# An attention chunk's k^T v as two matmuls of 64 stationary columns instead of one of 128

## The chip, the core and the metric

The kernel runs on one core of a Trainium2 chip. The metric is the device time of one execution in microseconds; the time before is the median of three executions. The engines in the text are TensorE (PE, with its weight loads as PEld), VectorE (DVE), ScalarE (ACT), GpSimdE (POOL) and the queues that issue DMAs (SP above all).

## The reference: what is computed

Three layers follow one another, on a batch of 4, 8 heads, 768 tokens and a head width of 48, all in fp32. The first is an attention with a decaying state, a 48 x 48 matrix for each head:

```
for t in range(S):
    state = alpha[:, :, t, :, None] * state + np.einsum('bhd,bhe->bhde', k[:, :, t], v[:, :, t])
    y[:, :, t] = np.einsum('bhd,bhde->bhe', q[:, :, t], state)
```

Then a token mixer and a channel mixer (`h = relu(x^T w_tok1) w_tok2`, `u = x + h^T`, `h2 = relu(u w_ch1) w_ch2`, result `u + h2`), and last a second channel mix with a receptance gate (`k = relu(xk w_k)`, `v = k*k w_v`, result `sigmoid(xr w_r) * v`).

## The kernel before

The attention is done in chunks of 128 tokens. A batch has 6 chunks and 4 pairs of heads, so 24 attention steps; the two heads of a pair lie in partitions 0 to 63 and 64 to 127, 48 of each 64 in use. In a step, TensorE transposes q, k and alpha (`transposes`, L500); VectorE scans alpha to the running product `decay` and to `suffix`, and scales q and k by them (`scans`, `scale_qk`); ScalarE and VectorE split the scaled operands into a high and a low part; TensorE transposes the scaled k (L514) and multiplies k by q for the scores (L518 in the first round, L522 later); VectorE masks the scores (`mask`, L922). `attention_out` then makes the chunk's output `y_ps` from the masked scores and v (L538), adds the part that comes from the state (L541), and, in all chunks but the last, computes k^T v into `kv_ps` (L544). ScalarE takes `y_ps` out (`high_x`, L745), and VectorE's `outputs` writes the new state from `kv_ps` (L939 in the first chunk, L941 later), and then the low part of x (L944). GpSimdE multiplies the old state by the chunk's whole decay (`carry_state`, L421).

The state of a pair is one tile of 128 x 96: head 0's 48 x 48 in its upper left part, head 1's in its lower right one, and zeros elsewhere (set once by a memset), so that one matmul (L541) serves both heads. v is kept zero padded in the same way: `vt3[vb][:, p, h, :]` has 96 columns, head h's 48 in their place and 48 of zeros. `kv_ps` is columns 128 to 223 of the PSUM bank in which `y_ps` has columns 0 to 95.

A matmul of fp32 operands is carried out as two pairs of instructions, each a weight load and a matmul (in the trace, a `matmul` of fp32 stands twice); a matmul of operands of type fp32r is one pair. The k^T v is of fp32; the mixer's matmuls (L617, L633) are of fp32r, three of them for each product.

Around the attention the work runs in rounds. Round 0 has only the attention of batch 0, in a pipeline of three steps' depth, beside the loading and splitting of the mixers' weights on ScalarE and GpSimdE. Rounds 1 to 3 (a loop on each engine) have 28 slots each: the attention of batch r, and interleaved with it, in the order of the code, the mixers of batch r - 1: two slots for the first token matmul, two for the second, then 24 channel-mixer units of nine L617 and nine L633 matmuls. In slot s `attention_out` is done for step s - 2, so slots 2 to 21 have a k^T v each, the last 18 of them beside a channel-mixer unit. After them come the mixers of batch 3 alone and the last layer. There is no scheduler: each engine executes its instructions in the order in which they are written, and semaphores hold it back. `y_done` tells ScalarE that a step's `attention_out` is through, `xhi_ready` tells VectorE that ScalarE has taken y, `state_ready` goes to GpSimdE and to TensorE's next chunk.

Of the kernel before, what the change touches and what calls it, by code (L numbers as in the profile page):

```python
# [13 lines left out]
def attention_mixer_channel_mix(nc, q, k, v, alpha, w_tok1, w_tok2, w_ch1, w_ch2,  # L14
# [4 lines left out]
    ALU = mybir.AluOpType  # L19
# [3 lines left out]
    B, H, S, D = q.shape  # L23
# [6 lines left out]
    DP = 64  # L30
# [21 lines left out]
    with ctx:  # L52
        def sb(name, shape, dt=F32):
            return ctx.enter_context(nc.sbuf_tensor(name, shape, dt))
# [29 lines left out]
        def wr_w(n, kt):  # L84
# [23 lines left out]
        kdt = relu_k[:, :, 2 * P:3 * P]  # L108
        state = sb("state", [P, NP, W2])
        state_d = sb("state_d", [P, 4, W2])  # L110
# [14 lines left out]
             for half, o in ((0, 0), (0, H * DP), (1, 0))]]  # L125
        qbd = free_words[1][:, H * DP:H * DP + 4 * P].rearrange("p (n t) -> p n t", n=2)
        vt3 = vt + [mixed[:, :, :].rearrange("p a t -> p (a t)")[:, 0:NP * 2 * W2]
                    .rearrange("p (a h e) -> p a h e", a=NP, h=2)]
# [24 lines left out]
        def y_kv(r, i):  # L153

            b_y = bank[6] if is_first(r) and i % 2 else bank[2]
            return b_y[:, 0:W2], b_y[:, P:P + W2]
# [100 lines left out]
        def chunk_buffer(r, c):  # L257


            if is_first(r):  # L260
                return c % 3, c // 3 + 1
            return c % 2, NC // 2 * (r - 1) + c // 2 + 1 + NC // 3
# [4 lines left out]
        def step(i):  # L267
            return i // NP, i % NP
# [115 lines left out]
        def _(pool):  # L384
# [24 lines left out]
            def split_lo(n):  # L409

                _, dst, off = PIECES[n]
                rows, cols = piece_size(n)
                pool.wait_ge(w_hi_ready, n + 1)
                nc.gpsimd.tensor_tensor(dst[1][:, off:off + rows * cols], staging(n)[0],
                                        dst[0][:, off:off + rows * cols], ALU.subtract).then_inc(w_lo_ready, 1)
# [34 lines left out]
            for n in range(NEARLY, NMIX):  # L450

                _, dst, off = PIECES[n]
                rows, cols = piece_size(n)
                raw, loaded, value = staging(n)
                pool.wait_ge(loaded, value)
                nc.gpsimd.tensor_copy(dst[0][:, off:off + rows * cols], raw).then_inc(w_hi_ready, 1)
                split_lo(n)
# [19 lines left out]
        def _(pe):  # L477
            PASSES = ((0, 0), (0, 1), (1, 0))

            def v_pair(vb, p):  # L480

                return vt3[vb][:, p, :, :].rearrange("p h e -> p (h e)").rearrange(
                    "p (n d) -> p n d", d=D)[:, 0:4:3, :]

            def transposes(r, i):
                c, p = step(i)
                qb, loads = chunk_buffer(r, c)
                if is_first(r) and i == 0:
                    pe.wait_ge(consts_g, 5)
                    pe.wait_ge(pair_loaded, 48)  # L490
                if is_first(r) and i == 1:
                    pe.wait_ge(consts_g, 15)
                if i % NP == (1 if is_first(r) and i < NP else 0):
                    pe.wait_ge(qka_loaded[qb], 48 * loads)
                if not isinstance(r, int):
                    pe.wait_ge(kd_ready, STEPS * r + i)
                elif i >= 2:
                    pe.wait_ge(kd_ready, i - 1)
                for n, dst in enumerate(transposed_qka(r, i)):
                    mm = nc.tensor.transpose(  # L500
                        dst, qka3[qb][n][:, 2 * p:2 * p + 2, :].rearrange("p h d -> p (h d)"), ident[:, :])
                mm.then_inc(tr_done, 1)
# [22 lines left out]
            def attention_out(r, i):  # L525
                c, p = step(i)
                pe.wait_ge(am_ready, STEPS * r + i + 1)
                vb, loads = chunk_buffer(r, c)
                pe.wait_ge(v_loaded[vb], 32 * loads)
                y_ps, kv_ps = y_kv(r, i)  # L530
                if not isinstance(r, int):
                    pe.wait_ge(xlo_ready, STEPS * r + i)
                elif i >= 2:
                    pe.wait_ge(xlo_ready, i - 1)
                if c > 0:
                    pe.wait_ge(state_ready, NST * r + i - NP + 1)
                for h in range(2):
                    mm = nc.tensor.matmul(y_ps, am[:, i % 2, h * P:(h + 1) * P], vt3[vb][:, p, h, :],  # L538
                                          start=(h == 0), stop=(h == 1 and c == 0))
                if c > 0:  # L540
                    mm = nc.tensor.matmul(y_ps, qd[:, i % 4, :], state[:, p, :], start=False, stop=True)  # L541
                if c < NC - 1:
                    pe.wait_ge(kdt_ready, NST * r + i + 1)
                    mm = nc.tensor.matmul(kv_ps, kdt[:, i % 2, :],  # L544
                                          v_pair(vb, p),
                                          start=True, stop=True)
                mm.then_inc(y_done, 1)

            def attention_part(r, s):
                tr, sc, yo = steps_of(r, s)  # L550
                if not is_first(r) and yo is not None:
                    attention_out(r, yo)
                if sc is not None:
                    attention_scores(r, sc)
                if tr is not None:
                    transposes(r, tr)
                if is_first(r) and yo is not None:
                    attention_out(r, yo)
# [162 lines left out]
        def _(act):  # L721
            def split_hi(n):
                _, dst, off = PIECES[n]
                rows, cols = piece_size(n)
                raw, loaded, value = staging(n)
                act.wait_ge(loaded, value)
                nc.scalar.activation(dst[0][:, off:off + rows * cols], raw, ACT.Copy).then_inc(w_hi_ready, 1)
# [139 lines left out]
        def _(dve):  # L867
# [58 lines left out]
            def outputs(r, i):  # L926
                c, p = step(i)
                G = STEPS * r + i
                y_ps, kv_ps = y_kv(r, i)
                dve.wait_ge(xhi_ready, G + 1)  # L930
                if 0 < c < NC - 1:
                    dve.wait_ge(state_d_ready, NSP * r + i - NP + 1)
                if c < NC - 1:
                    for h in range(2):
                        lanes = slice(h * DP, (h + 1) * DP)
                        kv = kv_ps[lanes, h * D:(h + 1) * D]
                        own = state[lanes, p, h * D:(h + 1) * D]
                        if c == 0:
                            ins = nc.vector.tensor_copy(own, kv)  # L939
                        else:  # L940
                            ins = nc.vector.tensor_tensor(own, kv, state_d[lanes, i % 4, h * D:(h + 1) * D], ALU.add)  # L941
                    ins.then_inc(state_ready, 1)
                xs = slice(p * W2, (p + 1) * W2)
                nc.vector.tensor_tensor(x[1][:, c, xs], y_ps, x[0][:, c, xs], ALU.subtract).then_inc(xlo_ready, 1)  # L944

            def attention_part(r, s):
                tr, sc, yo = steps_of(r, s)
                if is_first(r):
                    if sc is not None:
                        mask(r, sc)  # L950
                elif yo is not None:
                    outputs(r, yo)
                if tr is not None:
                    scans(r, tr)
                    scale_qk(r, tr)
                if is_first(r):
                    if yo is not None:
                        outputs(r, yo)
                else:
                    if sc is not None:  # L960
                        mask(r, sc)
                    if tr is not None:
                        split_low(r, tr)
# [139 lines left out]
```

## Time and profile before

| | |
|---|---|
| time, median of 3 executions | 812.43 us (810.9 to 812.52) |
| span of the profiled execution | 811.5 us |
| PE, PEld busy | 779.0 us (96%), 765.0 us (94%) |
| DVE, ACT, POOL busy | 492.4 us (61%), 332.8 us (41%), 103.9 us (13%) |
| mean granted TensorE clock | 0.989 of full speed |

The profile describes one execution; its span goes from the first instruction to the last. PE's matmuls are pipelined, and the duration given for one is from its start to its modelled end, so that durations overlap: how fast a stream of matmuls runs is read from the distance between starts. The busy shares are means over stretches with different limits: round 0 (up to about 59 us), rounds 1 to 3 (to about 470 us) and the rest, in which the change has no part.

### The profile page before, as it was taken

Reading aid. Unit: us, or ns where it says so; the run is one execution under the profiler, and the core shown is the slowest. Engines: PE = TensorE matmul, PEld = TensorE weight load, DVE = VectorE, ACT = ScalarE, POOL = GpSimd, SP = SyncE. Lnnn points to the kernel's source line nnn. Section 1 sums busy time; section 2 is a strip of 40 time slices with the busy share of each in tenths; the row PEclk is TensorE's granted clock in tenths of the full one; section 3 lists DMA queues with packets and bytes.
Section 4 is the critical chain, followed back from the end, with each engine's and each line's share of the span. In section 5 each row is a group of like instructions: output and inputs, shape, how many; then the busy total and the mean of one; then the engine's idle time right before and its main releaser. Section 6 shows DMA issues by size and latency. Waiting matters only on the chain.

```text
span 811.5 us, 14781 instructions
## 1 busy us (share of the span) xinstructions
PE 779.0 (96%) x4864; PEld 765.0 (94%) x4864; DVE 492.4 (61%) x1463; ACT 332.8 (41%) x848; POOL 103.9 (13%) x146
## 2 busy tenths in 40 slices
PE   6998999999999999899999999999699999999998
PEld 5887999998899999899999999999699999999998
DVE  7987777872677776367787522224835744744751
ACT  4773434331333433143334213125445644743741
POOL 2564000201000110100020013003200000000000
PEclk9999999999999999999999999999899999999999
DMA  9973223330132232112232003200101101101000
GB/s 189 202 171 64 40 42 52 66 57 21 40 51 40 41 69 40 41 30 40 48 50 74 1 30 99 93 30 16 45 29 50 39 29 49 39 29 49 10 29 29
DMA packets 114895, 43.88 MB, mean 54 GB/s; under 512 B 102160, under 2 KB 112016, under 8 KB 114832
## 3 DMA queue, kind: packets, MB, share of 16 engines
q1 hardware_dynamic: 113680, 38.36, 22.8%
q0 software_dynamic: 1152, 4.72, 1.6%
q8 instruction: 35, 0.57, 0.3%
q14 instruction: 28, 0.23, 0.1%
HBM read 33.63 MB, written 9.44 MB: 53 GB/s over the span
## 4 chain that ended last, share of the span: by engine, by line
PE 81%; DVE 8%; issue 5%; ACT 3%; POOL 1%; SPq 1%; DMA 1%; DVEq 0%; ACTq 0%; POOLq 0%
PE bank L633 17%; PE bank L617 17%; PE bank L699 12%; PE bank L677 12%; PE bank L686 5%; PE bank L538 3%; PE bank L522 3%; PE bank L597 3%; PE bank L500 2%; PE bank L603 2%; PE bank L541 2%; PE bank L571 2%; PE bank L544 1%; ACT qs_hi L756 1%; DVE decay L893 1%
## 5 line engine op out<-in xcount | busy, mean ns | idle before, releaser
L756 ACT ACTIVATE qs_hi<-qd,rlast 64x128 fp32r<-64x128 f32 x144 | 57.6, 400 | 145.2 <-DVE qd L903 143.4
L969 DVE SCALAR_TENSOR_TENSOR hid_lo<-bank,hid_hi 128x384 fp32r<-128x384 f32 x96 | 53.1, 553 | 71.4 <-ACT hid_hi L765 71.4
L765 ACT ACTIVATE hid_hi<-bank 128x384 fp32r<-128x384 f32 x96 | 46.5, 485 | 71.7 <-PE bank L617 71.7
L912 DVE SCALAR_TENSOR_TENSOR qs_lo<-qd,rlast,qs_hi 64x128 fp32r<-64x128 f32 x144 | 57.3, 398 | 27.9 <-ACT qs_hi L756 25.6
L845 ACT ACTIVATE relu_k<-bank 128x384 f32<-128x384 f32 x64 | 31.5, 492 | 102.3 <-PE bank L677 77.4
L617 PE MATMUL bank<-u_hi,wch_hi 128*128 128x384 f32 x288 | 71.1, 355 | 0.0
L617 PE MATMUL bank<-u_lo,wch_hi 128*128 128x384 f32 x288 | 66.0, 336 | 0.0
L617 PE MATMUL bank<-u_hi,wch_lo 128*128 128x384 f32 x288 | 65.6, 335 | 0.0
L633 PE MATMUL bank<-hid_lo,wch_hi 128*128 128x384 f32 x288 | 65.5, 334 | 0.0
L633 PE MATMUL bank<-hid_hi,wch_hi 128*128 128x384 f32 x288 | 65.4, 334 | 0.0
L633 PE MATMUL bank<-hid_hi,wch_lo 128*128 128x384 f32 x288 | 65.4, 334 | 0.0
L1072 DVE TENSOR_TENSOR x_half<-bank,x_half 128x384 f32<-128x384 f32 x24 | 13.4, 558 | 77.2 <-PE bank L699 77.2
L1059 DVE TENSOR_TENSOR relu_k<-relu_k 128x384 f32<-128x384 f32 x64 | 43.4, 678 | 27.6 <-ACT relu_k L845 24.8
L421 POOL TENSOR_TENSOR state_d<-state,decay 128x96 f32<-128x96 f32 x64 | 21.9, 345 | 266.0 <-DVE decay L893 266.0
L745 ACT ACTIVATE x_hi<-bank 128x96 fp32r<-128x96 f32 x96 | 24.0, 250 | 73.2 <-PE bank L544 56.7
L500 PE MATMUL bank<-ident,qka 128*128 128x128 f32 x264 | 45.4, 283 | 8.0 <-POOL causal L401 4.1
L538 PE MATMUL bank<-vt,relu_k 128*128 128x96 f32 x352 | 51.8, 270 | 0.7 <-DVE relu_k L922 0.7
L677 PE MATMUL bank<-x_hi,wtok_hi 128*128 128x384 f32 x192 | 44.8, 341 | 7.5 <-ACT relu_k L845 7.5
L538 PEld LDWEIGHTS bank<-vt,relu_k 128*128 128x128 f32 x352 | 50.5, 192 | 1.6 <-DVE relu_k L922 1.6
L617 PEld LDWEIGHTS bank<-u_lo,wch_hi 128*128 128x128 f32 x288 | 51.6, 188 | 0.0
L617 PEld LDWEIGHTS bank<-u_hi,wch_lo 128*128 128x128 f32 x288 | 51.6, 188 | 0.0
L633 PEld LDWEIGHTS bank<-hid_hi,wch_hi 128*128 128x128 f32 x288 | 51.2, 188 | 0.1
(126 smaller groups left out, 1855.5 us busy)
## 6 DMA issues: line engine op xcount, KB each, us to landing
w_raw<-in_moe_w_ch SPq DMA_DIRECT2D x12, 384.0 KB, 4.1
x_scratch<-x_half POOLq DMA_DIRECT2D x8, 576.0 KB, 3.5
out<-x_half SPq DMA_DIRECT2D x24, 192.0 KB, 1.9
vt<-in_v SPq DMA_DIRECT2D x44, 96.0 KB, 2.4
qka<-in_q SPq DMA_DIRECT2D x21, 192.0 KB, 3.2
qka<-in_k SPq DMA_DIRECT2D x21, 192.0 KB, 4.0
qka<-in_alpha SPq DMA_DIRECT2D x21, 192.0 KB, 4.2
qka<-x_scratch SPq DMA_DIRECT2D x4, 577.5 KB, 3.9
```

Of the source, the lines that this page charges most:

```text
L500: mm = nc.tensor.transpose(dst, qka3[qb][n][:, 2 * p:2 * p + 2, :].rearrange("p h d -> p (h d)"), ident[:, :])
L538: mm = nc.tensor.matmul(y_ps, am[:, i % 2, h * P:(h + 1) * P], vt3[vb][:, p, h, :], start=(h == 0), stop=(h == 1 and c == 0))
L617: mm = nc.tensor.matmul(dst, ch1_w(a, n % KC, jj), u[c][:, n % KC, half * HT:(half + 1) * HT], start=(n == 0), stop=(n == 3 * KC - 1))
L633: mm = nc.tensor.matmul(b_acc[m][:, 0:HT], ch2_w(a, jj, m), hid[c][:, j % HJ, :], start=(jj == 0 and n == 0), stop=(jj == NJ - 1 and n == 2))
L677: mm = nc.tensor.matmul(dst, wk_w(a, n % KC, j), mix_out[0][c][:, half, n % KC, :], start=(n == 0), stop=(n == 3 * KC - 1))
L686: mm = nc.tensor.matmul(b_acc[m][:, 0:DM], mix_out[1][a][:, half, n % KC, m * P:(m + 1) * P], wr_w(c, n % KC), start=(n == 0), stop=(n == ...
L699: mm = nc.tensor.matmul(bank[m][:, 0:DM], k2[a][:, n % NF, m * P:(m + 1) * P], wv_w(c, n % NF), start=(n == 0), stop=(n == 3 * NF - 1))
L756: nc.scalar.activation(dst[lanes, h * P:(h + 1) * P], qd[lanes, i % 4, :], ACT.Copy, scale=rlast[lanes, i % 4:i % 4 + 1])\
L765: nc.scalar.activation(dst, b_ring[t % 2][:, 0:HT], func).then_inc(tile_hi, 1)
L912: nc.vector.scalar_tensor_tensor(qs[1][lanes, cols], qd[lanes, i % 4, :], rlast[lanes, i % 4:i % 4 + 1], qs[0][lanes, cols], ALU.mult, ALU ...
L969: ins = nc.vector.scalar_tensor_tensor(dst, src, 0.0, hi, ALU.max, ALU.subtract)
L1059: nc.vector.tensor_tensor(relu_k[:, j % 2, :], relu_k[:, j % 2, :], relu_k[:, j % 2, :], ALU.mult).then_inc(k2_ready, 1)
```

## The change

On TensorE the k^T v of a pair, one matmul with 128 stationary columns (both heads' k) and the 96 columns of v that hold values, becomes two matmuls. Each has the 64 stationary columns of one head, streams that head's zero padded 96 columns of v, and writes its half of the PSUM partitions. On VectorE the two instructions that copied each head's 64 x 48 part into the state become one on the whole 128 x 96 tile, since the other parts are now zeros. Nothing else changes: the semaphores and their counts, and the order of all else, stay.

```diff
-            def v_pair(vb, p):
-
-                return vt3[vb][:, p, :, :].rearrange("p h e -> p (h e)").rearrange(
-                    "p (n d) -> p n d", d=D)[:, 0:4:3, :]
-
...
                 if c < NC - 1:
                     pe.wait_ge(kdt_ready, NST * r + i + 1)
-                    mm = nc.tensor.matmul(kv_ps, kdt[:, i % 2, :],
-                                          v_pair(vb, p),
-                                          start=True, stop=True)
+                    for h in range(2):
+                        lanes = slice(h * DP, (h + 1) * DP)
+                        mm = nc.tensor.matmul(kv_ps[lanes, :], kdt[:, i % 2, lanes], vt3[vb][:, p, h, :],
+                                              start=True, stop=True)
                 mm.then_inc(y_done, 1)
...
                 if c < NC - 1:
-                    for h in range(2):
-                        lanes = slice(h * DP, (h + 1) * DP)
-                        kv = kv_ps[lanes, h * D:(h + 1) * D]
-                        own = state[lanes, p, h * D:(h + 1) * D]
-                        if c == 0:
-                            ins = nc.vector.tensor_copy(own, kv)
-                        else:
-                            ins = nc.vector.tensor_tensor(own, kv, state_d[lanes, i % 4, h * D:(h + 1) * D], ALU.add)
+                    if c == 0:
+                        ins = nc.vector.tensor_copy(state[:, p, :], kv_ps)
+                    else:
+                        ins = nc.vector.tensor_tensor(state[:, p, :], kv_ps, state_d[:, i % 4, :], ALU.add)
                     ins.then_inc(state_ready, 1)
```

TensorE, a slot of the loop of rounds 1 to 3, from the end of a channel-mixer unit to the next transposes; before (an fp32 matmul stands once here; `relu_k` is the storage of the transposed k and `vt` that of v):

```order
L633 MATMUL bank<-hid_lo,wch_hi 128x384 x3
L538 MATMUL bank<-vt,relu_k 128x96 x2
L541 MATMUL bank<-state,qd 128x96
L543 REGISTER_ALU
L544 MATMUL bank<-vt,relu_k 128x96
L506 REGISTER_ALU
L514 MATMUL bank<-ident,kd 128x128
```

and the same place now:

```order
L629 MATMUL bank<-hid_lo,wch_hi 128x384 x3
L533 MATMUL bank<-vt,relu_k 128x96 x2
L536 MATMUL bank<-state,qd 128x96
L538 REGISTER_ALU
L541 MATMUL bank<-vt,relu_k 64x96 x2
L501 REGISTER_ALU
L509 MATMUL bank<-ident,kd 128x128
```

One matmul of 128 stationary columns became two of 64, between two neighbours of 128; line numbers are smaller since the helper is gone.

VectorE, a step of round 0, from the scaling of k to the next scan; before:

```order
L905 TENSOR_TENSOR kd<-bank,suffix 128x128
L941 TENSOR_TENSOR state<-bank,state_d 64x48 x2
L944 TENSOR_TENSOR x_lo<-bank,x_hi 128x96
L922 COPY_PREDICATED relu_k<-causal,bank 128x256
L893 SCALAR_TENSOR_TENSOR decay<-bank,zeros 128x128
```

and now:

```order
L901 TENSOR_TENSOR kd<-bank,suffix 128x128
L933 TENSOR_TENSOR state<-bank,state_d 128x96
L936 TENSOR_TENSOR x_lo<-bank,x_hi 128x96
L918 COPY_PREDICATED relu_k<-causal,bank 128x256
L889 SCALAR_TENSOR_TENSOR decay<-bank,zeros 128x128
```

Two instructions of 64 x 48 became one of 128 x 96, of the same size as the one behind it.

## Rows read from the trace of the kernel before

**Rows 1.** The page: busy time, clock in 40 slices, chain by engine.
```profile
PE 779.0 (96%) x4864; PEld 765.0 (94%) x4864; DVE 492.4 (61%) x1463; ACT 332.8 (41%) x848; POOL 103.9 (13%) x146
...
PE 81%; DVE 8%; issue 5%; ACT 3%; POOL 1%; SPq 1%; DMA 1%; DVEq 0%; ACTq 0%; POOLq 0%
```

**Rows 2.** PE timeline, one slot of round 1: start us, us, engine, line, what.
```profile
157.99 0.58 PE L538 MATMUL bank<-vt,relu_k 128*128 128x96 f32 x4
...
159.33 0.49 PE L500 MATMUL bank<-ident,qka 128*128 128x128 f32 x3
159.57 0.77 PE L617 MATMUL bank<-u_hi,wch_hi 128*128 128x384 f32 x3
...
162.78 0.47 PE L538 MATMUL bank<-vt,relu_k 128*128 128x96 f32 x3
```

**Rows 3.** Chain of waits, 138 to 150 us: start us, us, what.
```profile
138.31 0.24 PE bank L544 x2
...
138.57 0.26 ACT x_hi L745
...
144.27 0.19 DVE state L941
...
149.27 0.62 PE bank L522 x3
```

**Rows 4.** Line L544 alone: count, duration ns min/median/max, first and last start.
```profile
L544 PE MATMUL bank<-vt,relu_k x152: 275/275/421, 12.8 to 443.1; 128*128 128x96 f32 x152
...
L544 PE MATMUL bank<-mixed,relu_k x8: 275/275/275, 28.9 to 34.8; 128*128 128x96 f32 x8
```

**Rows 5.** PE timeline around one k^T v of round 1.
```profile
153.19 0.58 PE L538 MATMUL bank<-vt,relu_k 128*128 128x96 f32 x4
153.60 0.39 PE L541 MATMUL bank<-state,qd 128*128 128x96 f32 x2
153.83 0.39 PE L544 MATMUL bank<-vt,relu_k 128*128 128x96 f32 x2
154.05 0.27 PE L514 MATMUL bank<-ident,kd 128*128 128x128 f32 x1
```

**Rows 6.** The weight loads at the same place.
```profile
153.52 0.30 PEld L541 LDWEIGHTS bank<-state,qd 128*128 128x128 f32 x2
153.74 0.30 PEld L544 LDWEIGHTS bank<-vt,relu_k 128*128 128x128 f32 x2
```

**Rows 7.** PE timeline, round 0: two fp32 matmuls of 256 columns, then three transposes.
```profile
27.38 0.27 PE L514 MATMUL bank<-ident,kd 128*128 128x128 f32 x1
27.49 0.60 PE L518 MATMUL bank<-x_half,kd 128*128 128x256 f32 x2
27.92 0.49 PE L500 MATMUL bank<-ident,x_half 128*128 128x128 f32 x3
28.25 0.25 PE L538 MATMUL bank<-mixed,relu_k 128*128 128x96 f32 x1
```

**Rows 8.** DVE timeline, one step of round 0.
```profile
28.36 0.41 DVE L941 TENSOR_TENSOR state<-bank,state_d 64x48 f32<-64x48 f32 x2
28.81 0.26 DVE L944 TENSOR_TENSOR x_lo<-bank,x_hi 128x96 fp32r<-128x96 f32 x1
...
30.39 0.41 DVE L941 TENSOR_TENSOR state<-bank,state_d 64x48 f32<-64x48 f32 x2
```

**Rows 9.** Chain of waits in round 0: first and last state, and a POOL piece.
```profile
16.24 0.04 DVE state L939
...
36.16 0.81 POOL wch_lo L414
...
52.77 0.19 DVE state L941
```

**Rows 10.** DVE timeline, the two slots of round 2 without a channel-mixer unit.
```profile
212.17 0.56 DVE L971 TENSOR_TENSOR u_lo<-bank,u_hi 128x384 fp32r<-128x384 f32 x1 [1.21 <-ACT u_hi L765]
212.65 0.41 DVE L939 COPY state<-bank 64x48 f32<-64x48 f32 x2
213.09 0.26 DVE L944 TENSOR_TENSOR x_lo<-bank,x_hi 128x96 fp32r<-128x96 f32 x1
...
219.75 0.41 DVE L939 COPY state<-bank 64x48 f32<-64x48 f32 x2
```

## The prediction, made before the changed kernel ran

> **What bounds the kernel now.** I read the page first. TensorE is 96% busy and holds 81% of the chain of work that ended last; VectorE has 8% of it [rows 1]. Those are means, so next I read stretches with the timeline. In rounds 1 to 3 a slot with a channel-mixer unit repeats every 4.79 us (L538 at 157.99 and again at 162.78), and TensorE starts one matmul after another in it [rows 2]: there every nanosecond added between two matmuls is paid. The chain shows the exceptions. Once a round, from 138.57 to 149.27 us in round 1, it leaves TensorE and runs over ScalarE and VectorE, until L522 goes on [rows 3]; TensorE idles at its end. The two slots ahead of the channel-mixer units are led by the hand-over TensorE, ScalarE, VectorE [rows 10]. In round 0 the chain lies mostly on VectorE, with pieces on GpSimdE in the middle, as at 36.16 us [rows 9]; a step takes 30.39 - 28.36 = 2.03 us [rows 8].
>
> The changed lines work from 12.8 to 443.1 us and 160 matmul records belong to them, so 80 k^T v [rows 4]: 20 in round 0 and 20 in each of rounds 1 to 3. Of the 20 of a round, 18 stand beside a channel-mixer unit; two of these lie in the stretch from 138.57 to 149.27 us (or its like in rounds 2 and 3), where VectorE leads and TensorE has time [rows 3]. That leaves 3 x 16 = 48 on TensorE's path.
>
> **What a k^T v costs TensorE now.** From the first L541 matmul (153.60) to L514 (154.05) there are four intervals in 0.45 us, 0.112 us each [rows 5]. What sets it? Two fp32 matmuls of 256 columns take 27.92 - 27.49 = 0.43 us, 0.215 each [rows 7], so 0.84 ns for a column and 0.081 us for 96: shorter than 0.112. I conclude that streams of 96 columns are paced by the loading of 128 stationary columns, not by the stream. From the second L541 to L514 it is three intervals, 0.335 us.
>
> **What it costs afterwards.** Four matmuls instead of two, each still streaming 96 columns, so 0.082 each, with a weight load half as wide, which I take to be hidden (half of the 0.112 or less). Then the matmul ahead of the first, and the first three of them, have 0.082 us each, and the last, with a load of 128 columns behind it, 0.112: 0.440 us. That is +0.105, if nothing else happens.
>
> Something else may: every matmul in this trace has a 128 x 128 stationary operand, and the change alternates with 128 x 64 ones, in and out again, 80 times. No row shows what that costs. The low end is nothing, or even a gain, if the two heads, which lie in different columns of the array, stream side by side: only three intervals of 0.082 and one of 0.112 remain, 0.358, or +0.02. The high end is that the array empties first: the whole 0.275 us duration of the matmul in flight [rows 4] and a load that hides under nothing. A load stands 0.08 us ahead of its matmul (153.52 to 153.60, and 153.74 to 153.83) [rows 5, 6]; I take 0.06 for 64 columns. Going in, 0.275 + 0.06 = 0.335; three of 0.082; going out, 0.275 + 0.083 = 0.358; sum 0.939, or +0.60.
>
> I take a value between, the nearest that rows give a mechanism for: the next load can't be pulled ahead over a change of shape, but waits only until the stream before it is through. In 0.082 + 0.06 = 0.142, inside 0.246, out 0.082 + 0.083 = 0.165: 0.553 against 0.335, **+0.22 us** for each k^T v.
>
> Here the Trainium skill speaks against the change: "TensorEngine Tiling (Array Packing)", Key Properties, says that changing the tiling mode drains TensorE, though changing the tile does not. No run here shows it; by that rule the sum would lie at my value or above it.
>
> **What VectorE gains.** The two 64 x 48 instructions take 28.81 - 28.36 = 0.45 us until the next one starts; the next is 128 x 96 from the same bank and takes 0.26 [rows 8]. The new instruction has that shape, so -0.19 us. It counts where VectorE leads:
> - Rounds 1 to 3: two states in the stretch of rows 3, two in the slots of rows 10, so 12 x 0.19 = -2.3 us. In the latter, `y_done` comes some tenths later, while VectorE still has L971 and ScalarE its u_hi; I count nothing for it, and at most 0.2 us for each of 6 at the high end.
> - Round 0: twelve steps of the chain have a state of VectorE (first at 16.24, last at 52.77); in seven GpSimdE's splitting of weights leads, which doesn't change [rows 9]. VectorE's step would fall from 2.03 to 1.84. But TensorE is not idle: a step has L518 0.43, three transposes 0.33, L514 0.11 [rows 7], L538 0.41, L541 and L544 0.22 each [rows 5], in all 1.72 us; with 0.22 more 1.94, so it becomes the bound. Gain 0.09 x 12 = -1.1 us.
>
> In all other slots VectorE's saving hides behind TensorE's channel-mixer matmuls. POOL's `carry_state` and the DMAs see the same order and semaphores; nothing new waits. `y_done`, on the last of the four matmuls, comes at worst some tenths later; ScalarE and VectorE have idle time there.
>
> **Sum.** 48 x 0.22 = +10.6; -2.3; -1.1: +7.2 us, so a span of 818.7. The median of the runs is 812.43 and the profiled span 811.5, 0.9 less; the forecast in the measure of the runs is **819.6 us**.
>
> **Rivals.** What this kernel's measurement can tell from no change is about 0.2%, 1.6 us: faster is below 810.8, slower above 814.0.
> - *Side by side, no price for the change of shape* (+0.02): 48 x 0.02 = 1.0, -2.3, and round 0 stays VectorE's at 1.84 a step, 12 x 0.19 = -2.3: -3.6, or 808.8. For it: the heads' columns and PSUM partitions are disjoint. Against: each head's high and low pass still follow one another, and each needs a load. The skill's "TensorE: Matmul & The Clock Gate", Part 3, says that matmuls in different column groups run concurrently, starting about 4 ns apart. No row here shows it; by that rule, alone, the time is this one.
> - *Side by side, but with the forecast's price at the two borders*: 0.142 + 0.164 + 0.165 = 0.471, +0.136. 48 x 0.136 = 6.5, -2.3, -2.0: +2.2, or 814.6.
> - *One after another, no price at the borders* (+0.105): 48 x 0.105 = 5.0, -2.3, -2.3: +0.4, or 812.9.
> - *The array empties at each border* (+0.60): 48 x 0.60 = 28.8; in round 0 TensorE's step becomes 1.72 + 0.60 = 2.32, +0.29 for all 20, 5.8; the late `y_done` 1.2; -2.3: +33.5, or 846. For it: nothing in the trace says that a matmul of another shape may enter behind one in flight.
>
> The first rival is the one on the other side. It decides where a k^T v costs TensorE less than 0.05 us more: below that VectorE's -4.6 us outweighs 48 x 0.05 by more than the measurement's uncertainty.
>
> **Chances.** Forecast 0.36; emptied array 0.22 (with the values between it and the forecast); side by side without price 0.20; one after another without price 0.12; side by side with price 0.10. The likeliest gives the time, 819.6; its own range, with a border price between 0.03 and 0.10 us, is 816 to 825. The range for 8 in 10 leaves out a little on either side: 808 to 847. Faster by over 0.2%: 0.22, the side-by-side case and a little of the next. Within 0.2%: 0.13. Slower: 0.65.
>
> **What would show it.** In the slot of rows 2 the distance from L538 to L538 should be 5.01 us instead of 4.79; the emptied array would show 5.39, side by side 4.81. From the second state matmul to the transpose of k I expect 0.55 instead of 0.335 us, with a gap ahead of the first and behind the last of the four, and their starts 0.08 apart; starts of the two heads within a few nanoseconds would show them side by side. VectorE's state should be 80 instructions of about 0.25 us in place of 160 of 0.2, and its step in round 0 down to 1.94, with VectorE now waiting for TensorE there. The forecast fails if the weight loads of 64 columns are not hidden or the shape change costs more than 0.1 us a border; it fails the other way if the heads overlap. It also fails if VectorE's new instruction takes as long as the two (0.41): then 3.4 us of gain are gone, and the forecast's case becomes 823.

## The result and the profile after

The changed kernel takes 824.78 us (median of 4 runs, 823.62 to 825.48), the kernel before in the same session 812.03 us (810.9 to 812.52). The ratio is 1.0156, with a 95% interval of 1.014 to 1.0172: slower by 12.7 us. The forecast was 819.6 us, slower by 7.2; the direction held, and the time lies at the upper edge of the forecast's own range (816 to 825).

The page of the changed kernel, busy time and chain, answers to [rows 1]:

```profile
PE 794.0 (96%) x5024; PEld 765.9 (93%) x5024; DVE 479.8 (58%) x1383; ACT 332.6 (40%) x848; POOL 104.0 (13%) x146
...
PE 88%; DVE 4%; issue 4%; ACT 2%; DMA 1%; SPq 1%; DVEq 0%; ACTq 0%
```

TensorE has 160 pairs of instructions more, VectorE 80 instructions less, and VectorE's share of the chain went from 8% to 4%. The span is 823.5 us instead of 811.5.

The PE timeline of one slot of round 1 (start us, us, engine, line, what), against [rows 2, 5]:

```profile
157.29 0.58 PE L533 MATMUL bank<-vt,relu_k 128*128 128x96 f32 x4
157.71 0.39 PE L536 MATMUL bank<-state,qd 128*128 128x96 f32 x2
158.03 0.39 PE L541 MATMUL bank<-vt,relu_k 128*64 128x96 f32 x4
158.34 0.33 PE L509 MATMUL bank<-ident,kd 128*128 128x128 f32 x1
158.43 0.36 PE L517 MATMUL bank<-qs_hi,ks_hi 128*128 128x256 f32 x1
...
162.33 0.58 PE L533 MATMUL bank<-vt,relu_k 128*128 128x96 f32 x4
```

The slot has become 162.33 - 157.29 = 5.04 us long, from 4.79. From the first state matmul to the transpose of k it is 0.63 us (157.71 to 158.34) instead of 0.45, and the score matmul follows the transpose after 0.09 instead of 0.03: +0.18 and +0.06 make the +0.24. The 128*64 in the third row is the new stationary shape.

A narrow window of the same timeline shows how the four matmuls of a k^T v stand to each other:

```profile
157.82 0.28 PE L536 MATMUL bank<-state,qd 128*128 128x96 f32 x1
158.03 0.30 PE L541 MATMUL bank<-vt,relu_k 128*64 128x96 f32 x2
```

By 158.10 two of the four have started, both ended within 0.30 us. In the trace's single records the four start at 0, 7, 134 and 140 ns: two and two nearly at once. The first comes 0.205 us after the matmul ahead of it, where two matmuls of equal shape are 0.112 apart; the transpose comes 0.177 us after the last. The weight loads of the same place show why there is a gap:

```profile
157.63 0.30 PEld L536 LDWEIGHTS bank<-state,qd 128*128 128x128 f32 x2
158.03 0.20 PEld L541 LDWEIGHTS bank<-vt,relu_k 128*64 128x64 f32 x4
158.34 0.14 PEld L509 LDWEIGHTS bank<-ident,kd 128*128 128x128 f32 x1
```

Before, the loads of L541 and L544 stood 0.08 us ahead of their matmuls and under the matmul before [rows 5, 6]. Now the first load of the new shape starts at 158.03, when its matmul is shown to start too, 0.20 us after the last matmul of the old shape (157.82); and the first load of 128 columns after them, at 158.34, comes 0.17 us after the last of the four.

In round 0, the chain of waits of the changed kernel consists of TensorE alone, where it was VectorE [rows 9]:

```profile
35.83 0.73 PE bank L578 x3
36.56 0.11 PE bank L509
36.67 0.43 PE bank L513 x2
...
37.85 0.22 PE bank L536 x2
38.07 0.32 PE bank L541 x4
38.39 0.26 PE bank L509
```

The first row is the early token matmuls of batch 0, three of 384 columns, which stand in every fourth step. The chain gives them 0.73 us; by the starts of the k^T v they add 0.58 us to a step (2.56 against 1.98).

VectorE's state of one step of round 0 in the changed kernel, against [rows 8]:

```profile
30.22 0.26 DVE L933 TENSOR_TENSOR state<-bank,state_d 128x96 f32<-128x96 f32 x1
30.40 0.25 DVE L936 TENSOR_TENSOR x_lo<-bank,x_hi 128x96 fp32r<-128x96 f32 x1
...
32.24 0.26 DVE L933 TENSOR_TENSOR state<-bank,state_d 128x96 f32<-128x96 f32 x1
```

The new instruction lasts 0.26 us, but the next one starts 0.18 us after it (30.22 to 30.40), where it was 0.45 before. Yet the step is 32.24 - 30.22 = 2.02 us.

Where the 12.0 us of the span went, from the starts of the k^T v in the timelines of both kernels:

| stretch | before | changed | difference |
|---|---|---|---|
| start to the first k^T v | 12.80 | 12.37 | -0.4 |
| first to last of round 0 | 38.26 | 40.00 | +1.7 |
| to the first of round 1 | 23.29 | 23.89 | +0.6 |
| first to last in rounds 1, 2, 3 | 93.88, 93.86, 93.86 | 96.87, 96.84, 96.87 | +9.0 |
| between the rounds (two turns) | 43.63, 43.37 | 44.53, 43.12 | +0.7 |
| last to the end | 368.6 | 369.0 | +0.4 |

The rounds of one kernel differ by 0.03 us among each other. The other stretches are less steady. The +1.7 of round 0 is made of 1.1 us in its last twelve steps and of a first step of 3.14 instead of 2.48 us, against which stands the earlier start; from the start of the span, the last k^T v of round 0 comes at 52.4 instead of 51.1 us, +1.3. Three experiments below whose round 0 is that of the kernel before have it at 51.2 to 51.7 us, and TensorE's part alone at 52.3.

VectorE jumps back to the start of its loop once between two rounds. Its first instruction there has become late:

```profile
200.38 0.56 DVE L969 SCALAR_TENSOR_TENSOR h_lo<-bank,h_hi 128x384 fp32r<-128x384 f32 x1 [2.01 <-issue]
```

```profile
206.07 0.56 DVE L961 SCALAR_TENSOR_TENSOR h_lo<-bank,h_hi 128x384 fp32r<-128x384 f32 x1 [2.64 <-issue]
```

The first row is from the kernel before. At the second turn the idle interval is 1.88 us before and 2.60 now. TensorE waits for it at the next transpose of k: 1.18 and 1.33 us there, 0.70 and 0.68 before.

### The profile page after: what moved, and what is told of

It is laid out like the page before. It is cut to its first block, busy times and chain, and to the rows that moved or that the text cites. A ratio compares the mean times of both kernels' runs of the same rounds, so it can differ in the third digit from the quotient of the medians.

```text
span 823.5 us, 15021 instructions
## 1 busy us (share of the span) xinstructions
PE 794.0 (96%) x5024; PEld 765.9 (93%) x5024; DVE 479.8 (58%) x1383; ACT 332.6 (40%) x848; POOL 104.0 (13%) x146
## 4 chain that ended last, share of the span: by engine, by line
PE 88%; DVE 4%; issue 4%; ACT 2%; DMA 1%; SPq 1%; DVEq 0%; ACTq 0%
PE bank L629 17%; PE bank L613 17%; PE bank L695 12%; PE bank L673 12%; PE bank L682 5%; PE bank L533 4%; PE bank L495 3%; PE bank L593 3%; PE bank L517 3%; PE bank L541 3%; PE bank L599 2%; PE bank L509 2%; PE bank L536 2%; PE bank L567 2%; PE bank L513 1%
## 5 line engine op out<-in xcount | busy, mean ns | idle before, releaser
L533 PE MATMUL bank<-vt,relu_k 128*128 128x96 f32 x352 | 51.4, 268 | 0.1
L629 PEld LDWEIGHTS bank<-hid_hi,wch_hi 128*128 128x128 f32 x288 | 51.2, 188 | 0.1
L629 PEld LDWEIGHTS bank<-hid_hi,wch_lo 128*128 128x128 f32 x288 | 51.3, 188 | 0.0
```

The source lines that it names most:

```text
L629: mm = nc.tensor.matmul(b_acc[m][:, 0:HT], ch2_w(a, jj, m), hid[c][:, j % HJ, :], start=(jj == 0 and n == 0), stop=(jj == NJ - 1 and n == 2))
```

## The experiments

Two numbers are compared throughout, both from the timelines: the distance from the first to the last k^T v of a round in the loops (before 93.87 us), and four steps of round 0, in which the pattern repeats (before 2.03 + 2.03 + 2.30 + 1.77 = 8.13 us; changed 3 x 1.98 + 2.56 = 8.50).

**One head only.** The price of the border or of the number of instructions? The kernel before, with one matmul of 64 stationary columns; head 1's product and state are left out.

```diff
-                    mm = nc.tensor.matmul(kv_ps, kdt[:, i % 2, :],
-                                          v_pair(vb, p),
-                                          start=True, stop=True)
+                    for h in range(1):
+                        lanes = slice(h * DP, (h + 1) * DP)
+                        mm = nc.tensor.matmul(kv_ps[lanes, :], kdt[:, i % 2, lanes], vt3[vb][:, p, h, :],
+                                              start=True, stop=True)
...
-                    for h in range(2):
+                    for h in range(1):
                         lanes = slice(h * DP, (h + 1) * DP)
                         kv = kv_ps[lanes, h * D:(h + 1) * D]
```

> Only head 0's k^T v is made (one matmul of 64 stationary columns, one 64 x 48 state instruction); head 1's state stays zero. It has as many load and matmul pairs as the kernel before, in the changed shape. Theory 'border' (the price is the change of stationary shape, 0.09 us going in and 0.12 us going out, and the second head runs beside the first for nothing): the slot of rounds 1 to 3 stays at 5.02 to 5.03 us, as with both heads; the high and the low pass of the head start 0.127 us apart. Rival 'count' (the price is the doubled number of load and matmul pairs): the slot falls back to 4.79 us or a little less.

824.69 us in a single run. Its PE timeline:

```profile
157.03 0.58 PE L538 MATMUL bank<-vt,relu_k 128*128 128x96 f32 x4
157.45 0.39 PE L541 MATMUL bank<-state,qd 128*128 128x96 f32 x2
157.76 0.38 PE L546 MATMUL bank<-vt,relu_k 128*64 128x96 f32 x2
158.07 0.33 PE L514 MATMUL bank<-ident,kd 128*128 128x128 f32 x1
...
162.06 0.58 PE L538 MATMUL bank<-vt,relu_k 128*128 128x96 f32 x4
```

The same number of matmuls as in the kernel before, and the slot of the changed one: 162.06 - 157.03 = 5.03 us. From L541 to L514 it is 0.62 us; with both heads 0.63. In a window as narrow as above only one has started:

```profile
157.56 0.28 PE L541 MATMUL bank<-state,qd 128*128 128x96 f32 x1
157.76 0.30 PE L546 MATMUL bank<-vt,relu_k 128*64 128x96 f32 x1
```

The two passes of the head start 0.133 us apart (single records). So in the changed kernel it is the other head that starts 7 ns behind, and it costs 7 ns. The theory "count" is refuted: with no matmul more than before, all of the price is there.

**Two full matmuls.** Twice the instructions without a change of shape.

```diff
-                    mm = nc.tensor.matmul(kv_ps, kdt[:, i % 2, :],
-                                          v_pair(vb, p),
-                                          start=True, stop=True)
+                    for h in range(2):
+                        mm = nc.tensor.matmul(kv_ps, kdt[:, i % 2, :], vt3[vb][:, p, h, :],
+                                              start=(h == 0), stop=(h == 1))
```

> k^T v as two matmuls of all 128 stationary columns, a head's zero padded v each, accumulated; VectorE as before. No change of shape. Theory 'border': the two added pairs cost 0.112 us each, as every 128-column pair beside them, so a slot of 4.79 + 0.22 = 5.02 us and about 48 x 0.22 = 10.7 us, plus up to 2.5 us in round 0, where TensorE has 0.3 us of room for a step: 822 to 826 us. Rival 'count': the same, 5.03 us; this run alone does not separate them, it gives the price that two more pairs have without a border.

823.7 us (823.02 to 823.92), ratio 1.0135 (1.0118 to 1.0151). The distance in a round is 97.28 us, four steps of round 0 8.40. From its PE timeline:

```profile
157.00 0.39 PE L541 MATMUL bank<-state,qd 128*128 128x96 f32 x2
157.22 0.61 PE L545 MATMUL bank<-vt,relu_k 128*128 128x96 f32 x4
157.67 0.27 PE L514 MATMUL bank<-ident,kd 128*128 128x128 f32 x1
157.70 0.36 PE L522 MATMUL bank<-qs_hi,ks_hi 128*128 128x256 f32 x1
```

Six matmuls in 0.67 us, 0.112 each, and no gap on either side. That two full matmuls cost as much as two borders (a slot of 5.01 against 5.03 us) is a coincidence of two sizes; by itself this run would have fitted either theory.

**Four borders instead of two.** Head 0's k^T v stands ahead of L533, head 1's behind L536.

```diff
+                if c < NC - 1:
+                    pe.wait_ge(kdt_ready, NST * r + i + 1)
+                    lanes = slice(0, DP)
+                    nc.tensor.matmul(kv_ps[lanes, :], kdt[:, i % 2, lanes], vt3[vb][:, p, 0, :],
+                                     start=True, stop=True)
                 for h in range(2):
                     mm = nc.tensor.matmul(y_ps, am[:, i % 2, h * P:(h + 1) * P], vt3[vb][:, p, h, :],
...
-                    pe.wait_ge(kdt_ready, NST * r + i + 1)
-                    for h in range(2):
-                        lanes = slice(h * DP, (h + 1) * DP)
-                        mm = nc.tensor.matmul(kv_ps[lanes, :], kdt[:, i % 2, lanes], vt3[vb][:, p, h, :],
-                                              start=True, stop=True)
+                    lanes = slice(DP, 2 * DP)
+                    mm = nc.tensor.matmul(kv_ps[lanes, :], kdt[:, i % 2, lanes], vt3[vb][:, p, 1, :],
+                                          start=True, stop=True)
```

> The changed kernel with head 0's k^T v moved ahead of the two L533 matmuls and head 1's left behind L536: four borders for each k^T v instead of two, and no heads side by side. Theory 'border': added to the slot of 5.03 us are 0.11 going in behind a 384-column stream, 0.127 for the second pass, 0.177 + 0.03 going out: about 5.46 us, and 54 x 0.43 = 23 us in the loops and up to 8 us in round 0: 845 to 857 us. Rival 'count': the number of pairs is that of the changed kernel, slot 5.03 us and 825 us.

865.19 us (863.58 to 865.88), ratio 1.0646 (1.0627 to 1.0665); 106.0 us in a round. The same instructions as in the changed kernel, 40 us slower:

```profile
167.79 0.69 PE L632 MATMUL bank<-hid_lo,wch_hi 128*128 128x384 f32 x3
168.40 0.38 PE L535 MATMUL bank<-vt,relu_k 128*64 128x96 f32 x2
168.71 0.69 PE L538 MATMUL bank<-vt,relu_k 128*128 128x96 f32 x4
169.23 0.39 PE L541 MATMUL bank<-state,qd 128*128 128x96 f32 x2
169.55 0.38 PE L544 MATMUL bank<-vt,relu_k 128*64 128x96 f32 x2
169.86 0.33 PE L509 MATMUL bank<-ident,kd 128*128 128x128 f32 x1
```

The next slot's L535 starts at 173.94: 5.54 us against 5.03. By single records the added 0.50 us is 0.094 going in behind a stream of 384 columns (0.268 instead of 0.174), 0.133 for the head's second pass, 0.177 to L538 and 0.105 more between its first two matmuls. Going in costs the same behind 384 columns as behind 96 (0.205 - 0.112 = 0.093): a long stream ahead hides nothing of it. The time is 8 us over the expected 857 at most. The rounds add 27.4 us to the changed kernel's (9.1 each) where 23 were expected, round 0 adds 9.7 (49.7 us from its first to its last k^T v) where at most 8 were, and some 3 us lie between the rounds, for which nothing was counted.

**TensorE's part alone.** The changed matmuls, VectorE's two 64 x 48 instructions as before:

```diff
-                    mm = nc.tensor.matmul(kv_ps, kdt[:, i % 2, :],
-                                          v_pair(vb, p),
-                                          start=True, stop=True)
+                    for h in range(2):
+                        lanes = slice(h * DP, (h + 1) * DP)
+                        mm = nc.tensor.matmul(kv_ps[lanes, :], kdt[:, i % 2, lanes], vt3[vb][:, p, h, :],
+                                              start=True, stop=True)
```

> TensorE's part alone: two matmuls of 64 stationary columns, VectorE's two 64 x 48 state instructions as before. If TensorE leads in the changed kernel nearly everywhere, VectorE's slower form costs little: 825 to 827 us. If VectorE's saving is worth the 3.4 us or more that the prediction gave it: 828 us or more.

822.37 us (822.18 to 824.75), ratio 1.0129 (1.0103 to 1.0154). This is below both expectations, and below the full change, though the intervals of the two overlap. The stretches that the change touches don't say that: 97.18 us in a round against 96.86, so VectorE's part saves 0.3 us a round, and four steps of round 0 take 8.50 us with it and without. The difference lies between: 22.7 us from round 0 to round 1 (changed: 23.9) and 42.5 at both turns (44.5 and 43.1). In the second turn both kernels have the full granted clock (1.00), and the 0.65 us between them is VectorE's late start in the loop: here it is idle for 1.93 and 1.94 us there, as in the kernel before. For the first turn and the way to round 1 the clock comes in as well (0.96 against 1.00 in the first turn). The windows view (PE, PEld, DVE, ACT, POOL busy, granted clock) of the same 11 us shows a part of it, first the changed kernel, then this one:

```profile
66.00:77.00 11.00, 10.06 (x54) 9.85 (x55) 6.11 (x16) 3.00 (x8) 5.16 (x4) 0.69 0.32 35
```

```profile
66.00:77.00 11.00, 10.09 (x62) 9.88 (x63) 7.30 (x20) 3.00 (x8) 5.14 (x4) 0.84 0.28 31
```

TensorE runs at the lower of its two clocks for longer after the 3.4 idle us that end at 66.9 us, and the window has 54 instead of 62 matmuls. These two executions differ in it; the kernels' matmuls are the same there.

**VectorE's part alone.** One matmul of 128 columns, one state instruction; the cross-head products, which the reference has not, go into the state with it.

```diff
-                    for h in range(2):
-                        lanes = slice(h * DP, (h + 1) * DP)
-                        kv = kv_ps[lanes, h * D:(h + 1) * D]
-                        own = state[lanes, p, h * D:(h + 1) * D]
-                        if c == 0:
-                            ins = nc.vector.tensor_copy(own, kv)
-                        else:
-                            ins = nc.vector.tensor_tensor(own, kv, state_d[lanes, i % 4, h * D:(h + 1) * D], ALU.add)
+                    if c == 0:
+                        ins = nc.vector.tensor_copy(state[:, p, :], kv_ps)
+                    else:
+                        ins = nc.vector.tensor_tensor(state[:, p, :], kv_ps, state_d[:, i % 4, :], ALU.add)
```

> VectorE's part alone: one matmul of 128 stationary columns as before, the state taken in one 128 x 96 instruction, cross-head products included (so the state's zero parts no longer are zero). The slot of rounds 1 to 3 stays at 4.79 us. VectorE saves 0.19 us where it leads: 12 times in the loops, 2.3 us; in round 0 its step falls from 2.03 to 1.85 us, where TensorE's 1.72 us plus a fourth of the 0.52 us of early token matmuls (L582) for a step, 1.85 us, now stops it: 2 to 3 us. In all 807 to 809 us. Rival: nothing of it shows, 812 us, since TensorE is 96% busy.

809.75 us (808.12 to 811.16), before 813.36 in the same comparison, ratio 0.996 (0.9948 to 0.9972). The saving is real, 3 to 4 us, a little less than expected: 93.06 us in a round, 0.8 less, and 7.51 us for four steps of round 0 instead of 8.13. At the two jumps of its loop VectorE loses some of it: it is idle there for 2.66 and 2.59 us, as in the changed kernel. TensorE's timeline there has no slack left:

```profile
28.73 0.60 PE L518 MATMUL bank<-x_half,kd 128*128 128x256 f32 x2
29.16 0.49 PE L500 MATMUL bank<-ident,qka 128*128 128x128 f32 x3
29.49 0.58 PE L538 MATMUL bank<-mixed,relu_k 128*128 128x96 f32 x4
29.91 0.39 PE L541 MATMUL bank<-state,qd 128*128 128x96 f32 x2
30.13 0.39 PE L544 MATMUL bank<-mixed,relu_k 128*128 128x96 f32 x2
30.35 0.27 PE L514 MATMUL bank<-ident,kd 128*128 128x128 f32 x1
30.46 0.60 PE L518 MATMUL bank<-x_half,kd 128*128 128x256 f32 x2
```

One step is 30.46 - 28.73 = 1.73 us, the sum that the prediction made from single rows.

**The change in rounds 1 to 3 alone.**

```diff
+                    if is_first(r):
+                        mm = nc.tensor.matmul(kv_ps, kdt[:, i % 2, :],
+                                              v_pair(vb, p),
+                                              start=True, stop=True)
+                    else:
+                        for h in range(2):
+                            lanes = slice(h * DP, (h + 1) * DP)
+                            mm = nc.tensor.matmul(kv_ps[lanes, :], kdt[:, i % 2, lanes], vt3[vb][:, p, h, :],
+                                                  start=True, stop=True)
...
+                    if is_first(r):
+                        for h in range(2):
...
+                    else:
+                        if c == 0:
+                            ins = nc.vector.tensor_copy(state[:, p, :], kv_ps)
```

> Both parts of the change in rounds 1 to 3 alone, round 0 as before. If round 0 costs 1.7 us (k^T v of its first to its last step: 40.0 us instead of 38.3), this is 823 us, 11 us over before. By my prediction's reckoning, in which round 0 gains 1.1 us, it would be 826 us.

823.43 us (822.7 to 825.32), ratio 1.0131 (1.0114 to 1.0148). 96.85 us in a round, as with the full change, and 8.13 us for four steps of round 0, as before. Against the kernel before, each in its own comparison, this is +10.7 us and the full change +12.7, so round 0 costs rather than gains, by some 2 us; the intervals of this and of the full change overlap, so the sign of round 0 rests on its steps (8.50 against 8.13).

**Without the early token matmuls.** In both kernels the products of chunks 1 to 4 are left out.

```diff
                 for k, (i, j) in enumerate(PASSES):
+                    if 0 < c < NC - 1:
+                        continue
                     mm = nc.tensor.matmul(b_ring[0][:, 0:HT], tok1_w(i, c, 0), x[j][:, c, :],
```

> The kernel before without the early token matmuls (L582) of chunks 1 to 4. Theory: VectorE leads round 0, so the distance from the first to the last k^T v of round 0 stays at 38.3 us within 0.5 us. Rival (TensorE leads it already): about 2 us less.

> The changed kernel without the early token matmuls (L578) of chunks 1 to 4. Theory: TensorE leads round 0 after the change, and these three matmuls of 0.174 us every fourth step are the 0.13 us a step that the prediction left out. The distance from the first to the last k^T v of round 0 falls from 40.0 us by 3 or 4 times 0.52 us, to about 38.2 us, 1.98 us a step. Rival (VectorE or GpSimdE leads it): it stays at 40.0 us.

Single runs, 813.3 and 822.19 us. From the first to the last k^T v of round 0 the kernel before takes 38.17 us (with them 38.26): VectorE leads. The changed one takes 38.66 (40.00): of the groups left out two fall into the distance, and where a step was 2.56 us it is now 1.98. In its timeline steps without them are equally long (41.87, 43.85, 45.83):

```profile
41.87 0.33 PE L509 MATMUL bank<-ident,kd 128*128 128x128 f32 x1
...
43.85 0.33 PE L509 MATMUL bank<-ident,kd 128*128 128x128 f32 x1
...
45.83 0.33 PE L509 MATMUL bank<-ident,kd 128*128 128x128 f32 x1
```

The expected 38.2 had counted three or four groups; the mechanism is shown, for the changed kernel and not for the one before.

**VectorE's outputs at a later place.** The VectorE part alone pointed to a gain without a change on TensorE: take the state off the chain where VectorE leads, by order. Both on the kernel before, in rounds 1 to 3: the call of `outputs` moved behind the mask, or to the end of the step.

```diff
-                elif yo is not None:
-                    outputs(r, yo)
...
                     if sc is not None:
                         mask(r, sc)
+                    if yo is not None:
+                        outputs(r, yo)
                     if tr is not None:
                         split_low(r, tr)
```

> The kernel before, both k^T v forms as before, with VectorE's outputs (state and low part of x) of rounds 1 to 3 moved behind the mask and ahead of split_low, into the 0.34 us in which VectorE waits for ScalarE's qs_hi. If VectorE's state instructions matter only where VectorE leads (the VectorE part alone saved 0.8 us a round there), moving them off that chain saves about 0.34 us each in the two slots without a channel-mixer unit and in the two of the stretch behind read_sums: 0.7 to 1.4 us a round, 2 to 4 us in all: 808 to 811 us. Rival: the wait for TensorE's scores, which the mask needs, holds the outputs back and with them the next slot: no gain or a loss.

```diff
                     if tr is not None:
                         split_low(r, tr)
+                    if yo is not None:
+                        outputs(r, yo)
```

> The same with outputs at the very end of the step, behind split_low: the whole 0.7 us leaves the chain to ks_lo, for which TensorE waits, but stands ahead of the next slot's low part. In the stretch behind read_sums the idle interval of 1.3 us should go (as far as TensorE's other work lets it); in the slots without a channel-mixer unit the next u_lo comes later and may give it back. 0.5 to 1.5 us a round: 808 to 811 us. Rival: the next slot's low part (u_lo, hid_lo) leads, and the loss there outweighs it: 813 us or more.

Behind the mask: 812.71 us (810.22 to 814.05, 12 runs), ratio 1.0 (0.9988 to 1.0013). The profile has 93.4 us in a round, 0.5 less, but over all runs no gain can be told. The two slots around the stretch of [rows 3] take 10.24 us instead of 10.89, and the first two slots of the round, ahead of the channel-mixer units, 11.22 instead of 10.88: part of it is given back there. No gain is what the rival had; whether by its mechanism is not shown. At the end: 874.24 us (873.45 to 874.45), ratio 1.076 (1.0744 to 1.0776), 112 us in a round. The waits of its TensorE (waited for: us in total, times, longest):

```profile
PE bank L538 <- DVE x_lo L944: 44.2, 55, 2.2
```

and its timeline:

```profile
110.42 0.32 PE L538 MATMUL bank<-vt,relu_k 128*128 128x96 f32 x1 [0.71 <-DVE x_lo L944]
```

I had looked at the next slot's low part as the danger. The one that came is L538, the next step's first use of the bank: it waits for x_lo, which now stood behind `split_low`, which waits for ScalarE. No version beats the kernel before while computing the reference: what the VectorE part gains needs the cross-head products to be zero, and the matmuls that make them zero cost more.

## Why the prediction was right, and what was missing

**Slower, since TensorE leads in the slots: right.** 0.24 us in every slot that TensorE leads (4.797 us on the mean before, 5.033 now), and 9.0 of the 12.0 us in the three rounds. The forecast had 8.3 for them (10.6 less 2.3).

**The price of a k^T v, +0.22: right in size, +0.24 measured, from other parts.** The prediction put together four streams one after another (+0.105) and a small price at the borders (+0.11). Measured is the opposite mix, and that the sum came out is luck: one term was too high and the other too low by nearly as much. The heads run side by side, so the inside costs almost nothing: 0.140 us from the first start to the fourth, where two full matmuls had 0.112. The borders cost 0.093 going in and 0.065 + 0.056 going out, 0.214. So the "side by side, with a price at the borders" rival, given a tenth, names the mechanism, and its price (+0.136 in all) was too low. The price was bracketed between nothing and the emptied array; that the whole duration of 0.275 us and a load are waited for is refuted (0.205 to the next start, not 0.335). On the draining rule of "TensorEngine Tiling (Array Packing)" in the Trainium skill the trace agrees: at each change of shape there is a gap, and between the two heads, of one shape at different columns, there is none. The gap is smaller than the 0.275 us that the trace shows for the matmul in flight, whose end is modelled, so how far the array empties is not shown. With the Trainium skill's "TensorE: Matmul & The Clock Gate", Part 3, on matmuls side by side, the trace agrees as well, with 7 ns between the two heads' starts where the page has about 4.

**Streams of 96 columns are paced by the load of 128: the number held, the cause is not shown.** With two full matmuls the added pairs are 0.112 us apart like the others. But with loads half as wide the forecast's 0.082 did not come about: a head's passes are 0.133 us apart. Why these take longer than either stream or load is open; no run separates it.

**VectorE's saving, 0.19 a step: right in size, wrong in one of its places.** From the state to the next instruction's start it is 0.18 us against 0.45, and VectorE's part alone is worth 3 to 4 us. Where it shows can be read from the 19 distances between the k^T v of round 1 (us):

| | before | VectorE's part | TensorE's part | changed |
|---|---|---|---|---|
| first two distances, ahead of the channel-mixer units | 10.88 | 10.54 | 10.93 | 10.93 |
| third distance | 4.94 | 4.93 | 5.02 | 5.04 |
| two distances around the stretch of [rows 3] | 10.89 | 10.44 | 10.79 | 10.44 |
| the 14 others | 67.16 | 67.16 | 70.46 | 70.46 |

In the stretch of [rows 3] the two savings came, 0.45 us for 0.38 booked. In the two slots ahead of the channel-mixer units, where 0.38 us were booked as well, VectorE's part alone has 0.34, and the changed kernel has none: with TensorE's addition these distances are 10.93 us, whichever form VectorE's instructions have. The prediction named the later `y_done` there and counted nothing for it; what was booked and did not come is 1.2 us in the three rounds. The idle interval of TensorE ahead of the scores, from L514 to L522, was 1.31 us before, is 0.82 with VectorE's part alone and 0.42 in the changed kernel:

```profile
147.96 0.27 PE L514 MATMUL bank<-ident,kd 128*128 128x128 f32 x1
149.27 0.39 PE L522 MATMUL bank<-qs_hi,ks_hi 128*128 128x256 f32 x1 [1.04 <-DVE ks_lo L916]
```

```profile
152.94 0.33 PE L509 MATMUL bank<-ident,kd 128*128 128x128 f32 x1
153.36 0.39 PE L517 MATMUL bank<-qs_hi,ks_hi 128*128 128x256 f32 x1
```

That slot takes 0.7 us less instead of 0.24 more. With the third distance, which grows by 0.1, this is why 17 slots beside channel-mixer units give 3.0 us in a round and not 4.1.

**Round 0, -1.1 us: wrong in sign, +1.7.** This is the step that failed, and with 2.8 us (2.4 if counted from the start of the span) the largest part of the 4.8 us between the forecast +7.2 and the +12.0 of the spans. The step was "in all 1.72 us; with 0.22 more 1.94, so it becomes the bound". 1.73 was measured and 1.98 with the change. But the sum for TensorE left out the early token matmuls (L582), 0.52 to 0.58 us in every fourth step. Before, they hid in the room of 0.3 us a step that TensorE had beside VectorE; with that room gone they come on top: 3 x 1.98 + 2.56 = 8.50 us against 8.13. The runs without them show it. With them in the sum the forecast of four steps would have been 4 x 1.94 + 0.55 = 8.31, a loss. The prediction also left out of the change seven steps that GpSimdE led; now TensorE leads them too.

**The rest: between the rounds, which the forecast took as unchanged.** The two turns together are 0.7 us longer. Three things make this up. Each turn holds the last k^T v of a round, 0.24 us more; the forecast has these in its 48. In each, VectorE's first instruction of the loop is 0.6 to 0.7 us later, for which the forecast had no term. And in the second turn TensorE has the full granted clock, where the kernel before has 0.96; two kernels that show both clocks take 1.2 us less with the full one (without the early token matmuls 42.4 against 43.6, with two full matmuls 42.6 against 43.8). That gives 2 x 0.24 + 2 x 0.65 - 1.2 = 0.6. The late start goes with VectorE's state instruction: all kernels with two of them in the loop are idle there for 1.9 to 2.1 us, all with one (one head only and four borders among them) for 2.6 to 2.7, and the kernel that has both forms, one in round 0 and one in the loop, for 2.0 and 2.2. Why is open; no run separates it. On the way to round 1 the changed kernel has a granted clock of 0.86 and the kernel before 0.93, and +0.6 us. What of this and of the +0.4 at the end belongs to the change stays open; over the whole span the mean granted clock is the same, 0.989 and 0.990.

## What to carry to other kernels

A matmul of another stationary shape between full ones has a price at both borders, here 0.21 us in all, which is the same for one head between them and for two. One packed pair doesn't pay for it. Many in a row may; no run here tests that. Splitting an instruction of the engine that leads, to save one on an engine that mostly waits, gains only in the stretches that the second one leads, and a sum for the leading engine needs everything it does in the period, also what comes only in every fourth step. A place without a changed line can still change, as VectorE's start of the loop did, so the profile after is to be read there too. Before a result is moved to a later place in an engine's order, look for the next writer of its buffer, not only for its readers.

## What the hardware showed that I had not expected

The border price is the same behind a stream of 384 columns (0.094 us) as behind one of 96 (0.093). Going out, a second load of the full shape is late too: L509 to L517 is 0.084 us instead of 0.028. Two heads, each with its own weight loads and its own stream of 96 columns, cost 7 ns more than one (slots of 5.03 us both). And four matmul records of two fp32 products can interleave by pairs, though the program writes one product after the other; which of the records belongs to which pass the trace doesn't say.
